# Sliding-window attention with adapters on one core: masks of rounds 2 to 7 carried by the score products, three load slots in place of four

## The reference

```
scores = q @ k^T / sqrt(64)
plain:   rel >= 0 and rel < 32
dilated: rel >= 0 and rel < 128 and rel % 4 == 0
scores = where(mask, scores, -1e9);  attn = softmax(scores);  x = attn @ v
logits = x @ w_gate;  the two largest -> weights w by softmax
out = x + sum over the two chosen e of  w_e * (x @ A[e]) @ B[e]
```

## Time and profile before

| what | value |
|---|---|
| median of 3 runs | 100.3 us (100.02 to 101.3) |
| the profiled execution's own time | 100.78 us |
| its span, first to last instruction | 99.0 us |
| PE busy | 81.1 us (82%) |
| ACT busy | 71.4 us (72%) |
| DVE busy | 62.4 us (63%) |
| POOL busy | 54.6 us (55%) |
| loads (queue q0) | 14.23 MB, 72.1% of the 16 DMA engines' span |
| granted TensorE clock, mean | 0.976 |

### The profile page before, as it was taken

One profiled execution on the slowest core, in us unless ns is written; L12 is line 12 of the kernel. 1 busy time (PEld: TensorE's weight loads), 2 busy tenths in 40 slices (PEclk: granted clock), 3 DMA queues, 4 the chain that ended last, 5 costly groups with the idle time before them and its releaser, 6 DMA issues.

```text
span 99.0 us, 3612 instructions
## 1 busy us (share of the span) xinstructions
PE 81.1 (82%) x1587; PEld 59.7 (60%) x1587; DVE 62.4 (63%) x138; ACT 71.4 (72%) x123; POOL 54.6 (55%) x73
## 2 busy tenths in 40 slices
PE   3999969878569989999897979999599988776500
PEld 2443556466446875789666868877487877564300
DVE  5770009506469189459735698779494999979810
ACT  5195692599848974896995689989389989957400
POOL 5999902862449044406941297098076463665820
PEclk9999999999999999999999999999999999999955
DMA  2999999999999999999999999999999996976894
GB/s 18 314 201 211 202 214 224 200 210 226 210 213 213 212 211 214 220 215 207 218 217 213 213 214 213 213 209 186 206 383 425 432 409 287 409 309 251 352 410 194
DMA packets 6095, 24.50 MB, mean 247 GB/s; under 512 B 832, under 2 KB 960, under 8 KB 5440
## 3 DMA queue, kind: packets, MB, share of 16 engines
q0 software_dynamic: 3920, 14.23, 72.1%
q1 hardware_dynamic: 2016, 9.77, 24.6%
q10 hardware_dynamic: 144, 0.28, 0.7%
HBM read 29.07 MB, written 9.44 MB: 389 GB/s over the span
## 4 chain that ended last, share of the span: by engine, by line
PE 45%; DMA 15%; ACT 15%; POOL 10%; DVE 6%; issue 5%; POOLq 0%
PE ps L213 37%; DMA in<-in_qkv_dram 15%; ACT p L351 8%; POOL in L273 7%; PE ps L414 5%; DVE x L390 3%; ACT xt L424 2%; PE ps L504 2%; ACT zs L472 2%; POOL x L559 1%; DVE x L551 1%; POOL xb L397 1%; ACT gn L523 1%; PE ps L438 1%; ACT th L491 1%
## 5 line engine op out<-in xcount | busy, mean ns | idle before, releaser
L397 POOL CAST xb<-x 128x1152 bf16<-128x1152 f32 (+1 forms) x16 | 18.3, 1143 | 25.6 <-DVE x L390 25.6
L351 ACT ACTIVATE p<-ps 128x960 bf16<-128x960 f32 (+1 forms) x32 | 27.6, 900 | 3.4 <-PE ps L213 3.2
L213 PE MATMUL ps<-in,p 128*64 128x130 bf16 (+1 forms) x416 | 21.5, 221 | 4.1 <-ACT p L351 2.9
L390 DVE TENSOR_TENSOR x<-ps,rec 128x1152 f32<-128x1152 f32 x16 | 21.7, 1357 | 0.5
L213 PEld LDWEIGHTS ps<-in,p 128*64 128x64 bf16 (+1 forms) x416 | 17.1, 104 | 7.5 <-ACT p L351 3.9
L551 DVE TENSOR_TENSOR x<-x,ps 128x1024 f32<-128x1024 f32 (+1 forms) x16 | 17.5, 1116 | 3.4 <-PE ps L213 3.4
L387 DVE RECIPROCAL rec<-ps 128x18 f32<-128x18 f32 x16 | 4.3, 270 | 17.7 <-PE ps L213 17.6
L499 POOL TENSOR_TENSOR gz<-zs,g 128x640 bf16<-128x640 f32 x7 | 8.9, 1275 | 9.4 <-DVE g L494 9.4
L213 PE MATMUL ps<-warm 128*128 128x512 f32 x22 | 12.4, 706 | 1.5 <-DVE warm L217 1.5
L213 PEld LDWEIGHTS ps<-in 64*64 64x64 bf16 x576 | 10.9, 106 | 2.7 <-issue 0.7
L213 PE MATMUL ps<-in 64*64 64x96 bf16 (+1 forms) x576 | 11.9, 201 | 0.5 <-issue 0.5
(11 more groups left out here) (55 smaller groups left out, 101.6 us busy)
## 6 DMA issues: line engine op xcount, KB each, us to landing
in<-in_qkv_dram POOLq DMA_DIRECT2D x5, 1152.0 KB, 23.2
out_dram<-x SPq DMA_DIRECT2D x5, 1152.0 KB, 7.6
in<-in_qkv_dram POOLq DMA_DIRECT2D x10, 292.5 KB, 24.0
in<-in_qkv_dram POOLq DMA_DIRECT2D x10, 288.0 KB, 8.2
out_dram<-x SPq DMA_DIRECT2D x5, 576.0 KB, 3.0
in<-in_qkv_dram POOLq DMA_DIRECT2D x10, 146.2 KB, 8.1
in<-in_qkv_dram POOLq DMA_DIRECT2D x2, 434.2 KB, 13.8
out_dram<-x SPq DMA_DIRECT2D x1, 320.0 KB, 3.4
```

Of the source, the lines that this page charges most:

```text
L213: return nc.tensor.matmul(o, lhsT=lhsT, rhs=rhs, start=start, stop=stop, skip_group_check=True)
L351: return [nc.scalar.activation(p[:, :, :].rearrange("p h (s c) -> p h s c", c=PER)[:, :, b0 : b0 + nb, 0:SEG], PS[:, k.at : k.at + 2, 0 : ...
L390: nm = add(f"N{tag}", "DVE", ("el", XG), lambda: [nc.vector.tensor_tensor(X[r][:, XG * g : XG * g + XG].rearrange("p (b i n) -> p b i n", ...
L397: add(f"B{tag}", "POOL", ("el", cut), lambda: [nc.gpsimd.tensor_copy(XB[r % 2][:, g, 0:cut], X[r][:, XG * g : XG * g + cut])], [nm] + free)
```

## The change

For rounds 2 to 7 the four mask matmuls of a part are gone. The products of these rounds contract over all 128 partitions: the other 64 partitions of a head's query and key columns hold constants (`sinks`), chosen so that their product is zero inside the window and a large negative number outside. For g = 1 one block cannot be written that way and another only in part, so a g = 1 part begins with two narrow mask matmuls over the whole array ("bands"), 96 columns wide in S1 and 16 wide in S0. Rounds 0 and 1 keep their mask matmuls.

Since a head's other half is now taken by constants, the two heads of a pair can no longer share columns: a slot grows from 9288 to 13896 columns, and there are three in place of four. A load of round r waits for round r - 3. The X tiles of rounds 6 and 7 lie in the slot of rounds 2 and 5. The constants are written once per slot, by 12 copies of 64 x 2304 (`f`, 11 on DVE and one on ACT), from a grid that DVE builds first (`cb`, `cf`, `cg`, `ch`). The constants' DMA `con` grows from 64 KB to 192 KB, `vz30` and `vz31` on ACT fall away, and `Lr` is issued as two DMAs of 64 partitions in place of one of 128. In the list of the order, loads L3 to L6 and Lw3 to Lw6 stand elsewhere; from the line with `S041` on nothing but those moved.

```diff
-SLOTS = 4
+SLOTS = 3
+ON_ACT = ((0, 0, 0),)
...
-QK_IN_ORDER = [[2 * VB, 2 * VB + QK]] * 2
-V_AT = [[VB, 0], [ROW, ROW + VB]]
+QK_IN_ORDER = [[2 * VB, 2 * VB + QK], [2 * VB + 2 * QK, 2 * VB + 3 * QK]]
+V_AT = [[VB, 0], [HI, HI + VB]]
+CROSSED, MASKED, SHORT = (2, 4), 6, 1
...
+SUNK = -4096.0
...
+                out = ((w < k) | (w - k >= W) | cut).astype(np.float64)
+                first, last = ((32, 0), (0, 32))[(b + pr) % 2]
+                st[first : first + 32, pr, b] = out[:, 0:32].T
+                st[last : last + 32, pr, b] = out[:, 64:SEG].T
+                m[first + np.arange(32), pr, b, np.arange(32)] = 1.0
+                own = np.linalg.solve(st[:, pr, b].T, out[:, 32:64])
+                m[:, pr, b, 32:64] = np.round(own)
...
-    X = [sb(f"x{r}", [128, 2 * XG], FP) for r in range(B)]
+    X = [sb(f"x{r}", [128, 2 * XG], FP) for r in range(B - 2)]
+    SPARE = IN[(B - 3) % SLOTS]
+    X += [SPARE[:, 4 * XG * i : 4 * XG * i + 4 * XG].bitcast(FP) if nc is not None else None for i in range(2)]
...
+    add("cb", "DVE", ("cp", 2304), lambda: [nc.vector.tensor_copy(grid(SINK[:, :]), pattern())], ["con"])
...
+                def fill(i=i, a=a, g=g, copy=None):
+                    rows = half(1 - a)
+                    v = IN[i][rows, QK_IN_ORDER[a][g] : QK_IN_ORDER[a][g] + QK]
+                    return [copy(v, SINK[rows, :])] if g else [copy(grid(v), pattern(rows))]
...
-            a = add(f"L{r}", "POOL", ("dma", 128, 8 * QK, 1), lambda: [nc.gpsimd.dma_start(
-                out=IN[r % SLOTS][:, 2 * VB : 2 * VB + 2 * QK].rearrange("p (j n) -> p j n", j=2),
-                in_=qkv[r].rearrange("a p n -> (a p) n")[:, 0 : 2 * (QK + PAD)].rearrange("p (j n) -> p j n", j=2)[:, :, 0:QK],
-            )], [d for d in free if d[0] == "S"])
+            a = add(f"L{r}", "POOL", ("dma", 128, 8 * QK, 2), lambda: [nc.gpsimd.dma_start(
+                out=IN[r % SLOTS][half(h), QK_IN_ORDER[h][0] : QK_IN_ORDER[h][0] + 2 * QK].rearrange("p (j n) -> p j n", j=2),
+                in_=qkv[r, h, :, 0 : 2 * (QK + PAD)].rearrange("p (j n) -> p j n", j=2)[:, :, 0:QK],
+            ) for h in range(2)], [d for d in free if d[0] == "S"])
...
+                if r >= 2:
+                    first = True
+                    if g:
+                        u, x, w = ((MASKED - b0, 0, 0), (SHORT, 4 * SEG, 80))[b0 == 0]
+                        for pr in range(2):
+                            mm(PS[:, k.at + pr, u * SEG + w : u * SEG + SEG], ident(), CON[:, x + w : x + SEG], True, False)
+                        first = False
+                    for j in range(nb):
+                        n = 64 if b0 + j == NB - 1 else 80 if g and b0 + j == SHORT else SEG
+                        for pr, a, c in tiles:
+                            q = QK_IN_ORDER[a][g] + pr * S + 64 * (b0 + j)
+                            done.append(mm(
+                                PS[half(c), k.at + pr, j * SEG : j * SEG + n],
+                                t[:, q + 2 * S : q + 2 * S + 64], t[:, q : q + n], first and j == 0, j == nb - 1,
+                            ))
+                    return done[-4:]
...
-S031@3 D12@2 E031 S030@0 D10@5 T21@7 E030 C21 A12 S131@3 B20 V30@0 A10 E131
-U2@7 T20@6 R30 N30 Cp2 B30 L6 Lw6 V31@3 Cd2 C20 Z02@7 Y02 Z12@1 R31
+S031@3 D12@2 E031 S030@0 D10@5 T21@7 E030 C21 A12 S131@3 L6 B20 Lw5 V30@0 A10 f111 E131
+U2@7 T20@6 R30 N30 Cp2 B30 V31@3 Lw6 Cd2 C20 Z02@7 Y02 Z12@1 R31
```

More of the change, by code:

```diff
@@ L254, in zeros, with pattern, grid @@
     def zeros(i, a):
-        at = ROW if a == 0 else 0
+        at = HI if a == 0 else 0
         return IN[i][half(a), at : at + 2 * VB].bitcast(U32)
+    def pattern(rows=slice(0, 128)):
+        return ONE[rows, 256:512].rearrange("p (m n) -> p m n", m=2).unsqueeze(2).to_broadcast([rows.stop - rows.start, 2, NB, 128])
+    def grid(t):
+        return t.rearrange("p (m s n) -> p m s n", m=2, n=128)
+    add("cb", "DVE", ("cp", 2304), lambda: [nc.vector.tensor_copy(grid(SINK[:, :]), pattern())], ["con"])
+    add("cf", "DVE", ("cp", 128), lambda: [nc.vector.tensor_copy(
+        SINK[:, GRID:].rearrange("p (r n) -> p r n", r=2)[:, :, 128:192], ONE[:, 512:640].rearrange("p (r n) -> p r n", r=2))], ["cb"])
+    add("cg", "DVE", ("cp", 128), lambda: [nc.vector.tensor_copy(
+        SINK[:, 0:GRID].rearrange("p (r n) -> p r n", r=2)[:, r, 128:384].rearrange("p (b n) -> p b n", b=2)[:, :, 32:64],
+        ONE[:, 640 + 64 * r : 704 + 64 * r].rearrange("p (b n) -> p b n", b=2)) for r in range(2)], ["cf"])
+    add("ch", "DVE", ("zero", 64), lambda: [nc.vector.memset(
+        SINK[:, GRID:].rearrange("p (r n) -> p r n", r=2)[:, :, 64 * MASKED : 64 * MASKED + 64].bitcast(U32), 0)], ["cg"])
+    sunk = {}
+    for i in range(SLOTS):
+        for a in range(2):
+            for g in range(2):
+                def fill(i=i, a=a, g=g, copy=None):
+                    rows = half(1 - a)
+                    v = IN[i][rows, QK_IN_ORDER[a][g] : QK_IN_ORDER[a][g] + QK]
+                    return [copy(v, SINK[rows, :])] if g else [copy(grid(v), pattern(rows))]
+                if (i, a, g) in ON_ACT:
+                    f = add(f"f{i}{a}{g}", "ACT", ("el", 2304), lambda fill=fill: fill(copy=nc.scalar.copy), ["con", "ch", "tab"])
+                else:
+                    f = add(f"f{i}{a}{g}", "DVE", ("cp", 2304), lambda fill=fill: fill(copy=nc.vector.tensor_copy), ["con", "ch"])
+                sunk.setdefault((i, g), []).append(f)
     for i in range(SLOTS):
@@ L346, in scores @@
                 return done[-4:]
[L348 removed]
+            s = add(f"S{part}{tag}", "PE", ("s", nb, (4 if r < 2 else 2 * g) + 4 * nb), scores,
+                    qk_ready[r, g] + ["con"] + cuts * g + (sunk[r % SLOTS, g] if r >= 2 else []), k)
             def exp(b0=b0, nb=nb, k=k):
@@ L554, in adapters @@
             if nk == 1:
-                y = (DY[1][:, :] if last else IN[0][:, 1024 * (r % 2) : 1024 * (r % 2) + 1024].bitcast(FP)) if nc is not None else None
-                dy = add(f"dy{r}", "ACT", ("el", 512), lambda k=k[1], y=y: [nc.scalar.copy(y, bank(k, k.size - 1))], [d2] + ([] if last else used[4]), k[1])
+                y = (DY[1][:, :] if last else SPARE[:, 8 * XG + 1024 * (r % 2) : 8 * XG + 1024 * (r % 2) + 1024].bitcast(FP)) if nc is not None else None
+                dy = add(f"dy{r}", "ACT", ("el", 512), lambda k=k[1], y=y: [nc.scalar.copy(y, bank(k, k.size - 1))], [d2] + ([] if last else used[B - 3]), k[1])
                 v = X[r][:, XG * g + 512 : XG * g + 1024] if nc is not None else None
```

67 lines of the change are left out of this document (44 added, 23 removed).

## The result

| | before | changed |
|---|---|---|
| median, same chip | 100.68 us (100.02 to 101.3, 4 runs) | 104.59 us (104.05 to 106.16, 4 runs) |
| profiled execution, and its span | 100.78 us, 99.0 us | 104.33 us, 102.5 us |
| PE, DVE, POOL, ACT busy | 81.1, 62.4, 54.6, 71.4 us | 82.5, 73.5, 58.4, 71.4 us |

The change made the kernel slower: the ratio is 1.039, with a 95% interval of 1.033 to 1.045.

What follows compares the result with a forecast made beforehand. It took PE's order and the load queue, running at the same pace, to bound the kernel. V51's 3.3 us plus 0.3 behind it gave 3.6: profiled 100.78 to 104.4, median 100.3 to 103.9, range 102.8 to 105.2.

Steps and rivals of the forecast that it cites:

- Lw5 behind L6: Load queue: Lw5 lands near 62.2 us in place of 56.5, so V51 starts 3.3 us later; the largest term.
- the larger `con`: Load queue at the start: 0.13 MB more, 0 to 0.6 us, taken as 0.3 on Lw5's landing.
- The later of two delays counts: At V51: PE's own lateness (62.0 at most) and Lw5's landing (62.2) do not add; V51 starts 3.3 us later.
- U2 1.3 us late: POOL: the cast B20 queues behind L6's wait for S131, making PE 1.3 us late from U2 on.
- The fills: Constant copies, mostly in DVE's gaps: 1.0 us each; the three ahead of m01 make it 0.8 late.
- my row: DVE's 544-column copy in 0.38 us, from which a 2304-column fill was put between that and 1.6 us.
- Rival 1: Fills overrun DVE's gaps or hold POOL's casts, so PE reaches V51 after Lw5: 106.2 us, chance 0.12.
- a fill took over 1.5 us: DVE: one of the prediction's signs of being wrong; it expected fills of about 1 us or less.
- Products two at a time: PE scores: full-height products pass two at a time, 0.045 us a 96-column slot, so removing masks gains nothing for a part.
- Rival 3: PE scores: full-height products still pass four at a time, gaining 0.19 a part: 102.1 us (0.08) or 97.7 (0.04).
- the 0.1 that the prediction named as a sign of its being wrong: PE: the prediction is wrong if score parts shrink by 0.1 us or more; it expected about the same length.
- Carried to the end: PE from V51 on: order unchanged and dense, so the shift, 3.3 + 0.3 = 3.6 us, is carried to the end.

Runs made afterwards that it cites:

- e4: Kernel before with one load moved, Lw5 issued behind L6, four slots and all masks kept: 104.1 us, ratio 1.033.
- e1: Changed kernel with only the order list edited: L6 back behind B30, Lw5 and B20 no longer behind it: 102.38 us, ratio 1.016.
- e10: Changed kernel with both orders back, each band as two 64-column matmuls, and F1's fillers as 32 matmuls of 128 columns: 100.99 us, ratio 1.0005.
- e2: Changed kernel with Lw5 put ahead of L6, the cast B20 still behind L6: 106.25 us, ratio 1.048.
- e3: Changed kernel with the cast B20 put ahead of L6, Lw5 still behind L6: 106.79 us, no ratio.
- e8: Kernel before without the mask matmuls of rows 2 to 7, those masks left out of the computation: 101.55 us, ratio 0.999.
- e9: Changed kernel with both orders back and the long filler F1 written as 48 matmuls of 64 columns: 102.01 us, ratio 1.007.
- e12: Changed kernel, its order kept, with the long filler F1 written as 48 matmuls of 64 columns: 104.09 us, ratio 1.033.
- e11: Kernel before with only the long filler F1 written as 48 matmuls of 64 columns: 102.62 us, ratio 1.018.

## Why the prediction was right

**Lw5 behind L6: right, 3.07 for 3.3.** The landing was put at 62.2 and came at 61.87; the 0.3 for the larger `con` is the difference, that DMA displaced no load. That this order alone suffices is shown by e4, that without it more than half of the loss goes by e1. e10 loses the rest too, but it has three edits.

**The later of two delays counts: right.** PE's own order would have had V51 at about 60.4 (S150 ended at 60.17 and an exponential lies between), 1.5 us late, well inside the load's 3; in e2, where the load is in time, it came at 60.06. e2 and e3 show each delay without the other.

**U2 1.3 us late: under-sized, 2.4.** Of the difference 0.7 is the late start of this execution, 0.25 L6's two issues at 1.29 in place of 1.05, and 0.25 the time from S131's end (43.16) to L6's start (43.52), where I took 0.1. The shadow hid it.

**The fills: the right delay for the wrong reason.** I took 1.0 us each and got m01 0.8 late; it was 0.83 late. But 0.7 of that is the start again. Three fills of 0.76 overrun the gap of 2.19 by 0.1, and in e1, which started early, m01 was at 34.53 against 34.38. The Trainium skill, "VectorE: DVE Perf Modes", the perf-mode tier table, was nearer than my row: its 693 ns for 2048 elements give an estimate of 0.8 us, which the trace's 0.76 bears out. (Three of 0.8 overrun the gap by 0.2, where the prediction said that this estimate leaves no delay.) Rival 1, dear fills, is out. The prediction called itself wrong if a fill took over 1.5 us, and one did, 1.69 beside a cast. DVE had idle time there (0.59 left in front of R11), so nothing came of it.

**Products two at a time: right.** Rival 3 falls with S170's 0.44 and e8. The size was off: I took nothing for a part without bands and S170 costs 0.10 more, since a block needs 0.055 a slot (0.44 over 8 slots) where I scaled to 0.045. S071 costs 0.15 more where I had 0.22. Of the parts behind V51, all but S060 together grew by 0.6, against 0.3 forecast. S060 shrank, from 0.71 to 0.43, by more than the 0.1 that the prediction named as a sign of its being wrong: in before a place of the queue (2241) lies in it, and its products take 0.58 there where 20 others take 0.38. With it the growth is 0.3, as forecast, but by luck.

**Carried to the end: right in sum, not in course.** The lag is 3.07 at V51, 2.55 at V61 (the 1.10 stop of the earlier trace rows is gone), 3.57 at V70, 3.3 at D70. What gave the 1.0 back between V61 and V70 is the g2 of 0.97 us shown above and the four taller parts there (0.17 and 0.25). g2 took 0.20 before, when it began 0.1 us ahead of the cast B60; now it begins 0.2 behind B60's start (74.71) and ends with it (75.86), and N61 and Z15 stand behind it, where PE idles 0.59. The prediction had no such term as g2.

**The sum.** 104.4 was forecast for the profiled execution, 104.33 measured. The large term, 3.3 of 3.6, is the mechanism forecast. That the rest came to the 0.3 of the sum is luck: behind V51's start a stop of 0.52 came, one of 1.10 (allowed for in the range alone) went, and 0.59 were lost behind g2. With both orders back I expected 101.3 and got 102.4.

## What to carry to other kernels

When a change frees a resource and takes another (here slots), ask first what the new wait holds up in an in-order queue: a load that moved behind one transfer cost 3 us, while 3 us less PE work (e8) bought nothing. Two delays that run side by side towards the same reader were here not a sum but a maximum, so undoing one of them may show nothing, and an experiment has to undo both. Before a gain or loss of 1 to 2 us in a long unrolled program is put down to an edit, look for stops that wait for nothing and count instructions: adding or removing some upstream moves them.

## What the runs showed of the hardware

**Instruction blocks.** Stops of 0.5 to 2.2 us on PE stand at queue positions a multiple of 256 apart, each behind a 16 KB transfer on the instruction queue that started 2.2 to 2.6 us before PE goes on, while loads keep the DMA engines full (share 1.05 from 31 to 62 us). The Trainium skill, "Runtime: NRT & Kernel Launch", Instruction fetch mechanics, has the 256-instruction blocks of 16 KB and calls their cost mostly hidden; here it was not, 1.98 us in V51 in e1. Each transfer starts only when PE has passed the last such place; why one then starts 100 instructions ahead of the next and another 2 is open.

**The clock.** The granted clock fell to 0.50, the lower of its two levels (1.2 GHz), for 3.4 us towards the end of an idle time of PE of 3.50 us (e3) and of 2.30 (e4), and shortly after a stop of 2.16 (e2) and of 2.00 (e9); it stayed at 1.00 behind 1.79 (changed kernel), 1.86 (e12) and e1's 1.98. In e3 V51 took 2.28 us in place of 1.34 for it.

**A small DVE product held by a cast.** The g2 above, two operands in SBUF and 40 columns, took 0.97 beside a POOL cast, and 0.20 in before. It isn't the change's doing: in 12 of the 14 traces, e4 and e11 of the old kernel among them, this g2 begins 0.06 to 0.23 us after B60, ends some 0.05 after it and takes 0.97 to 1.14; only in before and e8 it begins 0.1 ahead and takes 0.20. The Trainium skill, "GPSIMD Engine Reference", Specifications, states that POOL's SBUF interfaces are shared with VectorE and contended by instructions with two SBUF inputs, and these rows agree.
